# Last layer of a sparse-attention and expert kernel: tokens taken in the order "no expert, then expert by expert", by row gathers and scatters

## The reference

```python
# 1: attention, B=2, H=8, S=768, D=64: keys within a window of 16 and block maxima of 32; x is its output, 1536 x 512
# 2: experts: E=8, F=1024
do_compute = x @ w_skip > 0
out = x.copy()
xc = x[do_compute]
e_idx = argmax(xc @ w_gate, axis=1)          # gate_w: its softmax
for e in range(E):
    h = maximum(xc[e_idx == e] @ w1[e], 0.0)
    y[e_idx == e] = gate_w * (h @ w2[e])
out[do_compute] = xc + y
# 3: last layer, 512 -> 2048 -> 512, all tokens
h = out @ w_in
g = where(h >= 1, h, where(h <= -1, 0, (h + 1) ** 2 / 4))
return g @ w_out
```

## Time and profile before

| | us |
|---|---|
| median of 3 runs (lowest, highest) | 493.11 (491.24, 495.24) |
| the profiled execution's own time | 492.58 |
| its span, first to last instruction | 490.9 |
| TensorE / VectorE / ScalarE / GpSimd busy | 454.3 / 219.9 / 192.2 / 87.9 |
| mean granted TensorE clock, share of full | 0.976 |
| DMA moved | 67.27 MB, mean 137 GB/s |

### The profile page before, as it was taken

How to read it: one execution, slowest core, us unless ns; L and a number is a source line. 1 busy time by engine, 2 the same in 40 slices (tenths; PEclk the granted TensorE clock), 3 DMA queues, 4 the chain that set the end, 5 groups by cost and what they waited for, 6 DMA issues and landing times.

```text
span 490.9 us, 10535 instructions
## 1 busy us (share of the span) xinstructions
PE 454.3 (93%) x3902; PEld 342.9 (70%) x3902; DVE 219.9 (45%) x531; ACT 192.2 (39%) x407; POOL 87.9 (18%) x136
## 2 busy tenths in 40 slices
PE   6899998767999988789999999999999999999995
PEld 6777776633443533578888888888888888888884
DVE  5687777711223221435665555443314544333332
ACT  8565654001222211435545544433323344333332
POOL 6765553021443533100000000000000000000000
PEclk9899999788999999999999999999999999999998
DMA  8999998979976296190000100300000001000002
GB/s 228 228 307 340 271 288 281 364 276 395 391 263 246 79 388 269 42 406 28 0 3 0 41 3 1 128 0 0 0 21 21 0 29 57 0 0 0 0 0 85
DMA packets 30626, 67.27 MB, mean 137 GB/s; under 512 B 3400, under 2 KB 9552, under 8 KB 30592
## 3 DMA queue, kind: packets, MB, share of 16 engines
q1 hardware_dynamic: 28960, 64.49, 38.7%
q0 software_dynamic: 1344, 1.76, 1.1%
q10 hardware_dynamic: 288, 0.52, 0.3%
HBM read 60.03 MB, written 7.73 MB: 138 GB/s over the span
## 4 chain that ended last, share of the span: by engine, by line
PE 56%; DMA 1%; DVE 0%; issue 0%; ACT 0%; DVEq 0%; POOLq 0%; SPq 0%
PE bank L1390 9%; PE bank L1391 9%; PE bank L1392 9%; PE bank L1371 9%; PE bank L1369 9%; PE bank L1370 9%; PE bank L1353 1%; DMA xrow<-x_rows 1%; DMA x_rows<-y_out,sidx 0%; PE bank L1065 0%; DVE x_sb L1024 0%; DVE stage L1035 0%; ACT x_sb L710 0%; DVEq L323 0%; POOLq L323 0%
## 5 line engine op out<-in xcount | busy, mean ns | idle before, releaser
L1390 PE MATMUL bank<-w_r,ghi 128*128 128x512 f32 x192 | 76.7, 399 | 0.0
L1391 PE MATMUL bank<-w_r,ghi 128*128 128x512 f32 x192 | 75.9, 395 | 0.0
L1392 PE MATMUL bank<-w_r,glo 128*128 128x512 f32 x192 | 75.9, 395 | 0.0
L1369 PE MATMUL bank<-x_sb,w_r 128*128 (+1 forms) x192 | 75.2, 392 | 0.7 <-DVE x_sb L1024 0.7
L1371 PE MATMUL bank<-x_sb,w_r 128*128 (+1 forms) x192 | 75.8, 395 | 0.0
L1370 PE MATMUL bank<-x_sb,w_r 128*128 (+1 forms) x192 | 75.1, 391 | 0.0
L1044 DVE TENSOR_TENSOR act_g<-act_g,clipped 128x512 f32<-128x512 f32 x48 | 33.3, 693 | 77.3 <-ACT clipped L728 77.3
L727 ACT ACTIVATE act_g<-bank,minus_c 128x512 f32<-128x512 f32 x48 | 33.0, 688 | 87.1 <-DVE clipped L1042 87.1
L1046 DVE TENSOR_TENSOR glo<-act_g,ghi 128x512 fp32r<-128x512 f32 x48 | 33.2, 692 | 34.8 <-ACT ghi L731 34.8
L731 ACT ACTIVATE ghi<-act_g 128x512 fp32r<-128x512 f32 x48 | 30.3, 632 | 37.8 <-DVE act_g L1044 22.8
L1042 DVE TENSOR_SCALAR clipped<-bank 128x512 f32<-128x512 f32 x48 | 33.0, 687 | 26.6 <-PE bank L1371 26.6
(11 more groups left out here) (172 smaller groups left out, 577.5 us busy)
## 6 DMA issues: line engine op xcount, KB each, us to landing
w_f<-w SPq DMA_DIRECT2D x64, 512.0 KB, 8.6
v_sb<-vW SPq DMA_DIRECT2D x8, 585.0 KB, 7.1
w_f<-w_in SPq DMA_DIRECT2D x8, 512.0 KB, 10.8
w_f<-w_out SPq DMA_DIRECT2D x8, 512.0 KB, 11.5
k_raw<-kT SPq DMA_DIRECT2D x8, 400.0 KB, 7.1
q_sb<-qT SPq DMA_DIRECT2D x16, 192.0 KB, 9.2
x_rows<-x_pair SPq DMA_DIRECT2D x8, 384.0 KB, 5.3
out<-stage SPq DMA_DIRECT2D x12, 256.0 KB, 2.2
```

What stands on the lines that cost most here:

```text
L1369: mm(bank[f % 2][:, :], hi, x_hi, start=(c == 0), stop=False)
L1390: mm(bank[4 + i][:, :], hi, w_hi, start=(f == 0), stop=False)
L1391: mm(bank[4 + i][:, :], hi, w_lo, start=False, stop=False)
L1392: last = mm(bank[4 + i][:, :], lo, w_hi, start=False, stop=(f == F2C - 1))
```

## The change

- An order of all tokens is computed: first those without an expert, then expert by expert; `perm` holds for each place the row number. For it VectorE gets `place_first`, `place_dead`, `place_all`, `hot_rows`, `hot_groups` and two operations that read the result; TensorE gets `count_dead` after tile 0 and 12 matmuls before expert 4; GpSimd one iota.
- The last layer reads its rows by gathers through `perm` and writes its results by scatters through `perm`, all 12 and 12 issued by GpSimd; SyncE and ScalarE no longer do. `stage_free` stands for `out_stored` where the stage buffers are taken again.
- GpSimd gathers block 0's four row tiles after `perm` is set, `experts_done` is at 5 and the loop's scatters have landed; gathers 0 and 1 alternate with two scatters (of the last pair of tiles but one), and the last two scatters follow gather 3. It waits for these before block 1's rows.
- TensorE transposes row tiles 0 and 1 before the last `down` and 2 and 3 after it, before the last `add_parts`; the 22 and the 4 x 3 fillers go. ScalarE and VectorE do splits 0 and 1 before and 2 and 3 after the first block's rows.
- The second half of the last layer's weights waits for `experts_done` at 7 only, no longer for the scatters.
- Of the 10 weight units after attention 4 are issued at once (`GAP`), the other 6 after the fourth gather; SyncE waits there for `xg_in` at 32 and not 16. Ahead of the first tile TensorE has 12 fillers for 6.

```diff
+GAP = 4
...
-            for n in range(sum(EARLY), 6 * UNITS):
+            for n in range(sum(EARLY), sum(EARLY) + GAP):
                 load_early(n)
             for par in range(2):
-                sp.wait_ge(xg_in[par], 16)
+                sp.wait_ge(xg_in[par], 32)
+            for n in range(sum(EARLY) + GAP, 6 * UNITS):
+                load_early(n)
...
-            half = half_tiles(sp)
-            for par in range(2):
-                sp.wait_ge(y_scattered[par], 16 * half + 32)
-            for i in range(2):
-                sp.dma_start(first_rows(i), x_rows[i * P:(i + 1) * P, :]).then_inc(first_in[i], 16)
+            sp.wait_ge(experts_done, 7)
             for j in range(2 * UNITS, 4 * UNITS):
                 load_last(j)
...
+            def gather_rows(r, rows, done):
+                pool.indirect_dma_start(rows, None, x_rows[:, :], bass.IndirectOffsetOnAxis(ap=perm[:, r:r + 1], axis=0),
+                                        bounds_check=TOK - 1, oob_is_err=False).then_inc(done, 16)
+            pool.wait_ge(perm_set, 1)
+            pool.wait_ge(experts_done, 5)
+            for par in range(2):
+                pool.wait_ge(y_scattered[par], 16 * half)
+                passed(pool, pool_passed)
+            gather_rows(0, first_rows(0), first_in[0])
+            scatter(0)
+            gather_rows(1, first_rows(1), first_in[1])
+            scatter(1)
+            for i in range(2, SUBT):
+                gather_rows(i, first_rows(i), first_in[i])
+            for par in range(2):
                 scatter(par)
+            for par in range(2):
+                pool.wait_ge(y_scattered[par], 16 * half + 32)
+                passed(pool, pool_passed)
+            def load_rows(tb):
+                for i in range(SUBT):
+                    r = SUBT * tb + i
+                    pool.wait_ge(x2tr_done, r + 1)
+                    gather_rows(r, xrow[:, i % 2, :], xy_in[i % 2])
+            def store(tb):
+                if tb:
+                    pool.wait_ge(out_stored, 64 * tb)
+                    pool.sem_inc(stage_free, 1)
+                for i in range(SUBT):
+                    r = SUBT * tb + i
+                    pool.wait_ge((stage_a, stage_v)[i // 2], 2 * tb + i % 2 + 3)
+                    pool.indirect_dma_start(out[:, :], bass.IndirectOffsetOnAxis(ap=perm[:, r:r + 1], axis=0),
+                                            stage[:, i, :], None, bounds_check=TOK - 1, oob_is_err=False).then_inc(out_stored, 16)
+            for tb in range(NTB - 1):
+                load_rows(tb + 1)
+                store(tb)
+            store(NTB - 1)
...
-            with act.Fori(0, number - 1) as n:
+            with act.Fori(0, number - 2) as n:
                 copy_rows()
                 take_parts()
                 take_hidden()
+            copy_rows()
+            act.wait_ge(experts_done, 6)
+            for j in range(2):
+                split_hi(j)
             take_parts()
+            take_hidden()
+            for i in range(2):
+                x2_hi(0, i, first_bank(i))
+            take_parts()
+            for i in range(2, SUBT):
+                x2_hi(0, i, first_bank(i))
+            for j in range(2, 4):
                 split_hi(j)
...
+            def place_all():
+                dve.wait_ge(dead_mm, 1)
+                link(v.tensor_copy(dead_n[:, :], bank[3][:, BATCH * QT:BATCH * QT + 1]))
+                link(v.tensor_tensor(dead_rank[:, :], bank[3][:, 0:BATCH * QT], dead_bf[:, :], ALU.mult))
+                link(v.tensor_scalar(count_c[:, :], count_c[:, :], dead_n[:, 0:1], None, ALU.add))
+                link(v.tensor_tensor(first_t[:, :, :], one_bf[:, :, :, :].rearrange("p b t n -> p (b t) n"),
+                                     count_c[:, :].unsqueeze(1).to_broadcast([P, BATCH * QT, EXP]), ALU.mult))
+                link(v.tensor_reduce(pos[:, :], first_t[:, :, :], AX, ALU.add))
+                link(v.tensor_tensor(pos[:, :], pos[:, :], rank[:, :], ALU.add))
+                link(v.tensor_tensor(pos[:, :], pos[:, :], dead_rank[:, :], ALU.add))
+                link(v.tensor_scalar(pos_r[:, :], pos[:, :], 0.5 - P / 2, ROUND_P, ALU.add, ALU.add))
+                link(v.scalar_tensor_tensor(pos_m[:, :], pos_r[:, :], ROUND_P, pos[:, :], ALU.subtract, ALU.subtract))
+            def hot_rows(b):
+                of = slice(b * QT, (b + 1) * QT)
+                v.tensor_tensor(hot_p[:, of, :], pos_m[:, of].unsqueeze(2).to_broadcast([P, QT, P]),
+                                line_f[:, :].unsqueeze(1).to_broadcast([P, QT, P]), ALU.is_equal).then_inc(hot_p_done, 1)
...
+            place_first()
             dve.wait_ge(idx_done, 1)
...
             v.tensor_copy(gate_all[:, :], bank[1][:, 64:64 + NT])
+            place_dead()
             hidden()
             no_result()
             rows(0, 1)
             keep_rows(2, 0)
+            place_all()
             hidden()
             no_result()
             rows(1, 1)
             keep_rows(3, 1)
+            hot_rows(0)
+            hot_rows(1)
+            hot_groups()
...
-            for par in range(2):
-                result(par, half - 1)
-            for j in range(4):
-                split_lo(j)
+            dve.wait_ge(perm_mm, 1)
+            link(v.tensor_copy(pos_m[:, :], bank[3][:, PERM:PERM + BATCH * QT]))
+            v.scalar_tensor_tensor(perm[:, :], bank[3][:, PERM + BATCH * QT:PERM + 2 * BATCH * QT], float(P), pos_m[:, :],
+                                   ALU.mult, ALU.add).then_inc(perm_set, 1)
+            for par in range(2):
+                hidden()
+                dve.sem_inc(xs_set, 1)
+                result(par, half - 2)
+            split_lo(0)
+            result(0, half - 1)
+            split_lo(1)
             for i in range(SUBT):
-                x2_lo(0, i)
+                x2_lo(0, i, first_bank(i))
+            result(1, half - 1)
+            for j in range(2, 4):
+                split_lo(j)
...
-            keep_busy(6)
+            keep_busy(12)
...
+            def count_dead():
+                pe.wait_ge(dead_set, 1)
+                for t in range(BATCH * QT):
+                    left = BATCH * QT - t
+                    mm(bank[3][:, t + 1:BATCH * QT + 1], ones_bf[:, :], dead_bf[:, t:t + 1].to_broadcast([P, left]), start=(t == 0), stop=False, skip_group_check=True)
+                mm(bank[3][:, 0:BATCH * QT], upper_bf[:, :], dead_bf[:, :], start=False, stop=True, skip_group_check=True).then_inc(dead_mm, 1)
...
             for e in range(EXP):
+                if e == EXP // 2:
+                    pe.wait_ge(hot_p_done, 4)
+                    for t in range(BATCH * QT):
+                        last = mm(bank[3][:, PERM:PERM + 2 * BATCH * QT], hot_p[:, t, :], hot_pq[:, t, :, :].rearrange("p a n -> p (a n)"),
+                                  start=(t == 0), stop=(t == BATCH * QT - 1), skip_group_check=True)
+                    last.then_inc(perm_mm, 1)
                 pe.wait_ge(w1_in[e % SLOTS], 64 * fills(e))
                 tile(e, e - 1 if e else None)
+                if e == 0:
+                    count_dead()
...
             add_parts(False)
+            for i in range(2):
+                transpose_x2(None, i)
             take(pe, hT_set)
             for half in range(2):
                 down(EXP - 1, half)
+            for i in range(2, SUBT):
+                transpose_x2(None, i)
             add_parts(False)
...
-            keep_busy(22)
-            for i in range(SUBT):
-                transpose_x2(None, i)
-                keep_busy(3)
             pe.wait_ge(x2lo_done, SUBT + 2)
```

More of the change, by code:

```diff
@@ L36 @@
 RANKS, COUNTS, LOGITS = 136, 192, 128
+PERM = 64
 EXP = 8
@@ L54 @@
 ROUND = 1.5 * 2.0 ** 23 * TS
+ROUND_P = 1.5 * 2.0 ** 23 * P
 CHUNK = 1024
@@ L297, in sparse_attention_moe_kernel @@
     out_stored = sem("out_stored")
+    stage_free = sem("stage_free")
     def unit_at(j):
@@ L326, in _ @@
         def _(sp):
-            sp.sem_inc(out_stored, 64)
+            sp.sem_inc(stage_free, 1)
             def load_q(pair):
@@ L1336, in _ @@
                         tile(e, e)
-            add_parts(False)
-            take(pe, hT_set)
-            for half in range(2):
-                down(EXP - 1, half)
-            add_parts(False)
             def transpose_x2(tb, i):
                 if tb is None:
-                    r, rows = i, first_rows(i)
+                    r, rows, to = i, first_rows(i), first_bank(i)
                     pe.wait_ge(first_in[i], 16)
                 else:
-                    r, rows = SUBT * tb + (SUBT + i), xrow[:, i % 2, :]
+                    r, rows, to = SUBT * tb + (SUBT + i), xrow[:, i % 2, :], bank[2 + i % 2]
                     pe.wait_ge(xy_in[i % 2], 32 * tb + 16 * (i // 2 + 1))
@@ L1352, in transpose_x2 @@
                 for c in range(DC):
-                    last = nc.tensor.transpose(bank[2 + i % 2][:, c * P:(c + 1) * P], rows[:, c * P:(c + 1) * P], ident[:, :])
```

(10 more changed lines are left out.)

111 lines of the change are left out of this document (70 added, 41 removed).

## The result

| us | before | after |
|---|---|---|
| median of the runs beside each other (20 and 20) | 494.41 | 488.61 |
| profiled execution's own time | 492.58 | 489.26 |
| its span | 490.9 | 487.5 |
| mean granted TensorE clock | 0.976 | 0.98 |

The ratio is 0.9906, 95% interval 0.9882 to 0.993: 4.65 us faster (3.5 to 5.8), by 0.9%, where 10.5 us were forecast. The time lies inside the range, the direction is right, the size less than half. The profiled executions differ by 3.4 us of span. To see where that comes from I cut both traces at the same five events. There is one ReLU for each of the 18 expert tiles, so the third and the 18th mark the first tiles and the last.

A forecast was written before the change was run, and what follows sets the result against it. TensorE was taken to bound the kernel, its last-layer 270.7 us unchanged, leaving two edges. From 492.58 us, -5.5 + 0.7 - 9.7 + 4.0 = -10.5 gave 482.1 us, range 475.5 to 489.5 (8 in 10).

The forecast's parts named there:

- the two edges named: Where the chain leaves TensorE: the start of the experts, and the gap between the last expert matmuls and the last layer.
- Part 1 and 2: Start of the experts: held-back weights let the first gather land sooner, -5.5 us; computing the token order costs +0.7.
- Part 4: Last layer's rows and results by GpSimd: free except the last four stores, +4.0 us, bounds +3 and +6.
- The estimate beside it: End of the program: by the Trainium skill's transfer formula the last store lands at 493.9, the tail nearer +3.5 us.
- This part stays: Last layer, first matmul to last result copied out: 270.7 us of TensorE alone, no matmul removed, so no change.
- Part 3: Gap before the last layer: block 0's gathers need no expert result, first matmul at 205.3 for 215.03, -9.7 us.
- Rival C: Gap only half closes: gathers 1 to 3 meet 4 MB of weights, TensorE idles, clock falls; 487.5 us, 15%.
- rival E: More than the sum: TensorE's 2 us stalls on "issue", all under a full DMA queue, fall away; 476 us, 15%.
- A: GpSimd is the slow part: an indirect DMA's time goes by bytes, 2 KB rows take 4.1 us; 505 us, 5%.
- B: Gathers issued during VectorE's weight splits stand until the operation ends, 1.2 us at each of four; 486.9 us, 5%.
- D: The start gains nothing: the queue isn't drained by 97, or gathers fall behind under unbroken load; 487.6 us, 10%.

The follow-up runs named there:

- g1: The changed kernel, unaltered, run again as a control: 489.34 us, ratio 0.9977 to the kernel before.
- e4: The kernel before with only the held-back weights, the wait at 32 and twelve fillers, natural token order: 488.35 us, ratio 0.9873.
- e1: The changed kernel with the last block stored directly by SyncE, its 512 output rows left in the new order: 483.25 us, ratio 0.9789.
- f2: e1's kernel plus one more gather by GpSimd after the last result, which nobody reads: 497.39 us in a single run.
- e2: The changed kernel with the second half of the last layer's weights held until block 0's rows are transposed: 487.44 us, ratio 0.9871.
- f4: e2's kernel with each result bank of the last slice copied out when it is done, not after all four: 495.76 us, ratio 0.993.
- g3: f4's kernel with six fillers instead of twelve, in the new order: 483.82 us, ratio 0.988 to the kernel before.
- g2: f3's kernel with each result bank copied out when done, natural order: 484.51 us, ratio 0.9868 to the kernel before.
- e3: The changed kernel with GpSimd issuing all four of block 0's gathers ahead of the two scatters: 492.74 us, ratio 1.0008.
- f3: e4's kernel with six fillers, as before, instead of twelve: 492.87 us, ratio 0.9852 to the kernel before.
- g4: The kernel before plus one unused tile of 64 bytes per partition where the change put perm: 492.82 us, ratio 0.9967.
- f1: The changed kernel with all ten weight loads at once, the wait at 16 and six fillers, so the order alone: 504.63 us, ratio 1.0009.

## Why the prediction was wrong in size

**The edges were the right ones.** The last layer's matmuls stayed on the path, the time came from the two edges named, and the end gave some of it back. Start, order and gap together were forecast at -14.5 (-5.5 + 0.7 - 9.7) and measured at -13.7 (-6.87 + 0.75 - 7.56).

**Part 1 and 2: the mechanism as written, the size in part by luck.** The gather landed early, the fillers bound, the clock stayed up, the third up came 6.87 us earlier (6.9 written). That the two agree so closely is luck: the stall of 1.39 us in the second up was in no term, and the first up came 0.3 sooner and the order's matmuls took less (0.5 us for 0.8) than written. Of the 1.4 taken off for later waits 0.75 appeared, the order's work included, but that is the mildest value of the kernels with held weights: g1, the same kernel, had 1.7 there and e4 4.0. By the 18th ReLU e4 was 3.7 us ahead of the kernel before, where -5.5 was written; the rest of its 6.3 came later. The cover of the VectorE work held: its two large comparisons took 1.82 us, and 1.9 was counted.

**Part 4: the step that failed.** "2.7 more, less a little" was taken as the end of the program. Every piece before it was right: the first store 1.39 us after the last copies began (forecast 1.5), the four 1.28 apart, landing 2.7 after the last issue, in sum 7.85 us after the last matmul; that alone would be +2.8 on the tail of 5.05. What the sum did not have is GpSimd's DRAIN: the span ended 4.0 us after the landing, and 6.7 after the last issue began, where 2.7 was taken over from SyncE. Measured +6.8 for +4.0, above the bound of +6 too. e1 shows that the whole of it goes with GpSimd having the last stores, f2 that one indirect DMA at the end is enough for the DRAIN's part. The estimate beside it, a landing at 493.9, makes +3.0 and not the +3.5 written, and lacks the DRAIN too. The bound was too tight since it was made from SyncE's end, where the span ends 2.7 us after the last issue, and carried over to an engine that ends otherwise; the trace of before held GpSimd's own end of program, at 208, among its records, but in none of the views that I read. This step is 2.8 of the 5.9 us between the forecast and the measured -4.65.

**The last layer: a term missing.** "This part stays" was right of the matmuls and wrong by 1.4 us of their time: 48 slices, each some 0.03 longer. Nothing in the trace of before could show it.

**Part 3: the gap by 2.1 us.** Rival C's mechanism came true: gathers 1 to 3 each took 6.4 to 6.9 us among the loads, TensorE idled 4.7 us for the first of them and its clock fell. I had let the fourth gather carry that risk ("some loads now start at 198"). They started at 189.36, since after part 3 they waited for `experts_done` alone, and this is given while the last tile is still ahead. e2 prices it at 4.1 us: the stretch was forecast at 14.45 (24.15 - 9.7), and was 12.45 without the loads and 16.59 with them. That the gap missed by only 2.1 is because another thing went well: before's own stall inside the down projection at 191.8, 2.0 us and half the clock after it, is absent, as rival E had it. C's price of 487.5 is thus near the measured time in part by accident.

**The others.** A is false: indirect DMAs of 2 KB rows hold GpSimd 0.97 to 1.06 us, as the 512-byte ones did. B's mechanism is real and its price was too high: 1.29 and 1.60 us beside splits, 0.9 us for both, where 1.2 each at four was written. Both ended 0.9 us after the split; in f4 a gather began with 1.16 us of a split left and took 2.07. The trace of before did show it, against what the prediction says: the scatter at 203.70 ended 0.85 us after the split that was under way, and the first gather, 1.33 us and not 1.03, ended 0.92 after an operation of VectorE, though the changed kernel's first gather was issued within the like operation and took 1.05. D is false: from 97 to 99 us the DMA engines were idle, and the first gather landed in 2.8 us. E came true in part, the stall at 191.8 being gone, but its reading "all under a full DMA queue" was wrong for that one: from 192.6 until TensorE went on at 193.79 the DMA share was 0.16 and then 0. What ends such stalls is open.

The four terms named give back what was missing: 2.8 at the tail, 1.4 in the last layer and 2.1 in the gap, less the 1.3 that the start did better than forecast, are 5.0, and -10.5 + 5.0 = -5.5 is the sum of the stretches. That the timed runs say -4.65 is within their interval and the spread of the attention.

**The edit itself.** Held weights alone gain 6.3 us (e4), and the whole change 4.65 (and in g1 nothing that the interval shows). So the new order costs about what it brings: -7.6 at its gap, +6.8 and +1.4 behind it. The intervals don't part the two. With late loads and staggered copies the order reaches the level of the natural order with held weights and staggered copies (g3 and g2), and not more. The version to keep is the simpler one, g2. e1's 0.9789 leaves its last 512 rows in the new order, and is no candidate.

## What to carry to other kernels

Count the end of a program to the last engine's DRAIN, and not to the last landing: work that moves to another engine at the very end takes over that engine's way of ending (here 6.7 us from the start of the last issue by GpSimd to the end of the span, 2.7 by SyncE). When a transfer is freed of a wait, ask which small transfers it now starts among; a small one behind 4 MB takes twice its time, and moving it in its queue only changes who waits (e3). Try each half of a two-part change alone: here one half had as much gain as the whole.

## What was not expected of the hardware

- GpSimd's DRAIN ended 5.47 us after its last issue was over in all eight kernels that end on an indirect DMA of 2 KB rows, whether that had landed 3.8 us (after) or 2.6 us (f2) before. In the kernel before and the four others whose last one is a scatter of 512-byte rows in the middle (e4, f3, g2, g4) it was 3.51 us. In e1 GpSimd waited for the landing of its last stores first, and the DRAIN took 5.1 us from there, at 402.8, under the last layer.
- An indirect DMA issued while a weight split of VectorE was under way ended 0.84 to 0.92 us after the split: 1.29 and 1.60 us (after), 2.07 (f4), where 1.0 is usual. It was so in every such case of the 14 profiles but one, a gather that began together with its split (g3, 1.00 us), and one with 0.05 us of split left. With other operations of VectorE it was so at times only: 1.33 us for the first gather before, 1.05 for that after, under the same kind of operation.
- 64 bytes more ahead of the tiles per partition went with a slice of 24 matmuls of 5.60 us and not 5.56, in g4 and after, though not in f1.
- The clock fell with TensorE's idling: 4.7 us idle, and the next 4.7 us ran at 0.50, 1.2 GHz (down 3.64 us); 1.7 us idle in e2, and the same down ran in 1.92.
- An indirect DMA's time on GpSimd didn't go by bytes: 1.02 us for 64 KB, 0.97 for 256 KB. A 256 KB store by it landed in 2.7 us. By the Trainium skill (DMA: Bandwidth & Descriptors, Anatomy of one DMA), 2.0 us plus bytes over 436 GB/s, the estimate is 2.6, and the trace agrees.
